# Strassen's product with fifteen sums for the first product of two dense layers, in token groups of 768

## The reference, cut to what matters

```python
# attention with a decaying state: q, k, v are (2, 8, 768, 64)
for t in range(S):
    state = gamma * state + outer(k[t], v[t]);  y[t] = scale * q[t] @ state
x = y as (1536 tokens, 512)
h = x @ w_in                      # (512, 2048)
x = (h * sigmoid(1.702 * h)) @ w_out              # layer 1
xn = x / sqrt(mean(x * x) + 1e-6) * rms_g
x = (silu(xn @ w_gate) * (xn @ w_val)) @ w_out2   # layer 2, 1536 hidden features
```

## Time and profile before

| | us |
|---|---|
| median of 3 runs (lowest, highest) | 622.95 (622.73, 623.17) |
| span of the profiled execution | 621.5 |
| PE busy | 613.0 |
| DVE busy | 338.9 |
| ACT busy | 238.7 |
| POOL busy | 128.7 |

### The profile page before, as it was taken

One profiled execution on the slowest core, in us unless ns is written; L12 is line 12 of the kernel. 1 busy time (PEld: TensorE's weight loads), 2 busy tenths in 40 slices (PEclk: granted clock), 3 DMA queues, 4 the chain that ended last, 5 costly groups with the idle time before them and its releaser, 6 DMA issues.

```text
span 621.5 us, 8409 instructions
## 1 busy us (share of the span) xinstructions
PE 613.0 (99%) x3058; PEld 510.0 (82%) x3058; DVE 338.9 (55%) x463; ACT 238.7 (38%) x407; POOL 128.7 (21%) x98
## 2 busy tenths in 40 slices
PE   7999999999999999999999999999999999999997
PEld 7888888888888888888888888888888888888886
DVE  3665544546644447774446775444755554544443
ACT  1434544444444445444434333333333334332232
POOL 2642000003200006960004970001950000000000
PEclk9999999999999999999999999999999999999999
DMA  8897200000000002323230000001000000100001
GB/s 320 289 403 280 119 0 0 0 0 0 0 0 0 0 1 69 133 62 124 85 137 1 2 0 0 0 0 67 1 0 0 0 0 0 69 0 0 0 1 68
DMA packets 8560, 34.62 MB, mean 56 GB/s; under 512 B 992, under 2 KB 1120, under 8 KB 7520
## 3 DMA queue, kind: packets, MB, share of 16 engines
q1 hardware_dynamic: 8544, 34.42, 15.4%
HBM read 31.27 MB, written 3.15 MB: 55 GB/s over the span
## 4 chain that ended last, share of the span: by engine, by line
PE 95%; DMA 2%; issue 1%; POOL 0%; SPq 0%; DVE 0%; POOLq 0%
PE acc L311 37%; PE gate L311 37%; PE val L311 16%; DMA raw<-attn_in 2%; PE gate L279 1%; PE val L258 1%; PE acc L248 1%; PE gate L273 1%; PE gate L367 0%; PE gate L395 0%; POOL arena L719 0%; POOL arena L711 0%; DVE arena L696 0%; SPq L176 0%; SPq L174 0%
## 5 line engine op out<-in xcount | busy, mean ns | idle before, releaser
L467 ACT ACTIVATE sig<-gate 128x512 f32<-128x512 f32 x83 | 49.6, 597 | 215.6 <-PE val L311 126.8
L311 PE MATMUL gate<-x_hi,win_hi 128*128 128x512 f32 x336 | 130.8, 389 | 0.0
L311 PE MATMUL gate<-x_lo,win_hi 128*128 128x512 f32 x336 | 130.7, 389 | 0.0
L311 PE MATMUL gate<-x_hi,win_lo 128*128 128x512 f32 x336 | 130.7, 389 | 0.0
L625 DVE TENSOR_TENSOR g_lo<-g,g_hi 128x512 fp32r<-128x512 f32 x83 | 63.8, 768 | 58.0 <-ACT g_hi L472 58.0
L587 DVE TENSOR_TENSOR win_lo<-raw,win_hi 128x512 fp32r<-128x512 f32 (+1 forms) x84 | 86.9, 1035 | 11.2 <-ACT win_hi L423 11.2
L472 ACT ACTIVATE g_hi<-g 128x512 fp32r<-128x512 f32 x83 | 52.5, 633 | 96.9 <-DVE g L620 55.8
L593 DVE TENSOR_TENSOR wout_lo<-raw,wout_hi 128x512 fp32r<-128x512 f32 x84 | 69.2, 824 | 16.3 <-ACT wout_hi L427 15.9
L311 PE MATMUL acc<-g_hi,wout_hi 128*128 128x512 f32 x192 | 75.3, 392 | 0.0
L311 PE MATMUL acc<-g_lo,wout_hi 128*128 128x512 f32 x192 | 74.8, 389 | 0.0
L311 PE MATMUL acc<-g_hi,wout_lo 128*128 128x512 f32 x192 | 74.7, 389 | 0.0
(11 more groups left out here) (63 smaller groups left out, 728.1 us busy)
## 6 DMA issues: line engine op xcount, KB each, us to landing
raw<-attn_in SPq DMA_DIRECT2D x24, 512.0 KB, 7.3
raw<-w SPq DMA_DIRECT2D x12, 768.0 KB, 4.2
raw<-w SPq DMA_DIRECT2D x8, 1024.0 KB, 8.6
out<-arena SPq DMA_DIRECT2D x2, 1024.0 KB, 4.5
out<-arena SPq DMA_DIRECT2D x4, 256.0 KB, 2.1
arena<-tables SPq DMA_DIRECT2D x1, 518.0 KB, 5.5
arena<-tables SPq DMA_DIRECT2D x1, 256.0 KB, 7.8
ident<-ident_in SPq DMA_DIRECT2D x1, 64.0 KB, 9.8
```

The source lines that it names most:

```text
L311: mm = pe.matmul(out_ap, a, b, start=start and i == 0, stop=stop and i == len(pairs) - 1)
L467: act.activation(sig[par][:, :], gate[par][:, :], ACT.Sigmoid, scale=1.702 if layer == 1 else 1.0).then_inc(sig_done, 1)
```

## The change

The layers are rewritten; attention keeps its steps, but its output goes to `x32` in full float32, one buffer per batch row, and is split into upper and lower parts later.

- Tokens go in two groups of 768 in place of three blocks of 512. There are four phases: layer 1 for either group, then layer 2 for either group.
- The first product of a layer is taken for two hidden tiles (256 features) by 768 tokens by 512 input features at a time, as a 2 by 2 by 2 block product by Strassen's scheme with seven block products and fifteen sums (Winograd's form). A unit `hidden(p, j)` is seven products, each of 2 feature blocks by 3 passes, so 6 matmuls of 384 columns. Some sums are formed in PSUM by letting several products add into one bank; others by ACT copies and DVE additions (`copy_m1`, `copy_m5`, `copy_u2`, `c12`, `c22`).
- Product 4 of unit `n` adds to what `c22(n)` left, and is issued in the next unit behind that one's products 1 and 5 (`fourth`).
- POOL forms four sums of weight blocks for each unit (`weight_sums`), DVE four sums of input blocks for each phase (`sum_x`). Seven weight blocks and seven input blocks are then split, where four were before.
- All activated features of a group stay on chip (`g32`), and a stage after the hidden stage multiplies them by the second weights into eight banks of 384 columns (layer 1) or six of 512 (layer 2).
- Weights are loaded anew in each phase, 512 KB a unit, through three buffers `raw`.
- The sigmoid followed by a multiplication is replaced by one ACT function in layer 1 and by Silu in layer 2.
- The norm moves from POOL to ACT (squares), DVE (sums, diagonals, `normalise`) and PE, within the hidden stage of the phase that follows.
- The hardware loops are gone; all instructions are written out.

The core of the new code, in the order of engines PE, ACT, DVE, POOL (`lower_next(r, k)` on DVE and `split_next(r, k)` on ACT are parts 0, 1, 2 of the next unit's weights, of 768, 512 and 512 columns, or one part of 1024 for a projection unit; `gate_tile` is the product of Silu and value in layer 2; parts 0, 1 and 2 on ACT wait for 1, 2 and 4 of the unit's POOL sums):

```diff
+HALF = SEQ // 2
+OPERAND = 2 * HALF
+PHASES = ((1, 0), (1, 1), (2, 0), (2, 1))
+HIDDEN = {1: NF1 // 2, 2: NF2}
+PROJECT = {1: NF1 // 2, 2: NF2 // 2}
+SET = ((0, 1, 2), (3, 4, 5))
+FIRST = {1: (6, 7, 0, 1, 2, 4, 3, 5), 2: (6, 7, 0, 1, 2, 4)}
+FINAL = {1: (0, 1, 2, 3, 4, 5, 6, 7), 2: (0, 1, 2, 4, 6, 7)}
...
+def product(i, n, role, half, place, c, start):
+    p, j = hidden_units[n]
+    r = at["hidden", p, j]
+    q = (quad_at[r] + half) % 3
+    dst = bank[SET[n % 2][role]][:, 0:HALF]
+    if j == 0:
+        pe.wait_ge(x_lo_done, 7 * p + c + 1)
+    for kk in range(2):
+        w, x = cols(2 * place + kk, P), cols(2 * c + kk, HALF)
+        pe.matmul(dst, w_hi[q][:, w], x_hi[:, x], start=start and kk == 0, stop=False,
+                  skip_group_check=True)
+        pe.matmul(dst, w_hi[q][:, w], x_lo[:, x], start=False, stop=False, skip_group_check=True)
+        mm = pe.matmul(dst, w_lo[q][:, w], x_hi[:, x], start=False, stop=kk == 1, skip_group_check=True)
+    mm.then_inc(m_done[i], 1)
...
+def fourth(n):
+    pe.wait_ge(c22_done, n + 1)
+    product(4, n, 2, 1, 1, T4, False)
...
+def hidden(p, j):
+    n, r = h_at[p, j], at["hidden", p, j]
+    pe.wait_ge(w_lo_done, lo_at[r] + 1)
+    if n < 2:
+        when(pe, bank_free(n, 2))
+        pe.wait_ge(x_lo_done, 1)
+        pe.matmul(bank[SET[n][2]][:, 0:HALF], w_hi[quad_at[r] % 3][:, 0:P], x_hi[:, 0:HALF],
+                  start=True, stop=True, skip_group_check=True)
+    when(pe, bank_free(n, 0))
+    product(1, n, 0, 0, 1, B11, True)
+    when(pe, bank_free(n, 1))
+    product(5, n, 1, 0, 0, T1, True)
+    if j > 0:
+        fourth(n - 1)
+    pe.wait_ge(w_lo_done, lo_at[r] + 3)
+    pe.wait_ge(m1_copied, n + 1)
+    product(6, n, 2, 1, 2, T2, False)
+    product(2, n, 0, 0, 2, B21, False)
+    pe.wait_ge(m5_copied, n + 1)
+    product(3, n, 1, 1, 3, B22, False)
+    pe.wait_ge(u2_copied, n + 1)
+    product(7, n, 2, 1, 0, T3, False)
...
+def norm_bcast(i):
+    pe.wait_ge(mean_done, i + 1)
+    pe.wait_ge(diag_done, i + 1)
+    for th in range(2):
+        mm = pe.matmul(bank[6 + th][:, 0:HALF], ones[:, :], diag[:, cols(th, HALF)], start=True, stop=True)
+    mm.then_inc(bcast_done, 1)
...
+for p, (layer, _) in enumerate(PHASES):
+    for j in range(HIDDEN[layer]):
+        hidden(p, j)
+        if p in (1, 2) and j == 2:
+            norm_totals(p - 1)
+        if p in (1, 2) and j == 4:
+            norm_bcast(p - 1)
+    project_phase(p)
...
+def copy_m1(n):
+    act.wait_ge(m_done[1], n + 1)
+    when(act, bank_free(n, 2))
+    a, b = SET[n % 2][0], SET[n % 2][2]
+    act.activation(bank[b][:, 0:HALF], bank[a][:, 0:HALF], ACT.Copy).then_inc(m1_copied, 1)
...
+def squares(i, th):
+    if th == 0:
+        act.wait_ge(evac_act, evac_at[i + 1])
+        act.wait_ge(evac_dve, evac_at[i + 1])
+    if 2 * i + th > 0:
+        act.wait_ge(sum_sq_done, 2 * i + th)
+    for dh in range(2):
+        act.activation(square[dh][:, :], x32[i][:, cols(2 * dh + th, OPERAND)], ACT.Square)\
+           .then_inc(squared, 1)
...
+for c in (T1, T2, B22, T3, T4):
+    split_x(0, c)
+for p, (layer, _) in enumerate(PHASES):
+    for j in range(HIDDEN[layer]):
+        n, r = h_at[p, j], at["hidden", p, j]
+        if j > 0 and not is_val(n - 1):
+            activate(n - 1, 2)
+        copy_m1(n)
+        copy_m5(n)
+        if j > 0 and not is_val(n - 1):
+            activate(n - 1, 3)
+        split_next(r, 0)
+        copy_u2(n)
+        if not is_val(n):
+            activate(n, 0)
+        split_next(r, 1)
+        split_next(r, 2)
+        if not is_val(n):
+            activate(n, 1)
+        if p in (1, 2) and j < 2:
+            squares(p - 1, j)
+        if j == HIDDEN[layer] - 1:
+            split_g(p, 0)
+            split_g(p, 1)
+    for j in range(PROJECT[layer]):
+        n, r = h_at[p, HIDDEN[layer] - 1], at["project", p, j]
+        if j == 0 and not is_val(n):
+            activate(n, 2)
+        split_next(r, 0)
+        for f in (2 * j + 2, 2 * j + 3):
+            if f < TILES[layer]:
+                split_g(p, f)
+            if f == 2 and not is_val(n):
+                activate(n, 3)
+        if p < len(PHASES) - 1 and 1 <= j <= 4:
+            for c in ((B11, B21), (T1, T2), (B22, T3), (T4,))[j - 1]:
+                split_x(p + 1, c)
+        split_next(r, 1)
+        split_next(r, 2)
...
+def sum_x(i, c):
+    g = PHASES[i][1]
+    b11, b12, b21, b22 = (x_block(g, b) for b in (B11, T1, B21, B22))
+    if c == T1:
+        if i < 2:
+            dve.wait_ge(y_copied, 11 + i)
+        else:
+            dve.wait_ge(x_normed, 8 * (i - 1))
+        dve.wait_ge(x_lo_done, 7 * i + 1)
+        dve.tensor_tensor(t3[:, :], b22, b12, ALU.subtract).then_inc(x_sums, 1)
+        dve.tensor_tensor(b12, b12, b11, ALU.subtract).then_inc(x_sums, 1)
+    elif c == T2:
+        dve.wait_ge(x_sums, 4 * i + 2)
+        dve.tensor_tensor(b11, t3[:, :], b11, ALU.add).then_inc(x_sums, 1)
+    else:
+        dve.wait_ge(x_sums, 4 * i + 3)
+        dve.wait_ge(x_lo_done, 7 * i + 2)
+        dve.tensor_tensor(b21, b21, b11, ALU.subtract).then_inc(x_sums, 1)
...
+def c12(n):
+    b = bank[SET[n % 2][1]][:, 0:HALF]
+    dve.wait_ge(m_done[3], n + 1)
+    dve.wait_ge(u2_copied, n + 1)
+    dve.tensor_tensor(b, b, u2[n % 2], ALU.add).then_inc(c12_done, 1)
...
+def c22(n):
+    a, b = bank[SET[n % 2][0]][:, 0:HALF], bank[SET[n % 2][2]][:, 0:HALF]
+    dve.wait_ge(m_done[7], n + 1)
+    dve.wait_ge(m5_copied, n + 1)
+    dve.wait_ge(*taken(n, 1))
+    dve.tensor_tensor(a, b, m5[n % 2], ALU.add).then_inc(c22_done, 1)
...
+def add_squares(i, th):
+    dve.wait_ge(squared, 4 * i + 2 * th + 2)
+    dve.tensor_tensor(square[0][:, :], square[0][:, :], square[1][:, :], ALU.add).then_inc(sq_added, 1)
+    if i > 0 and th == 0:
+        dve.wait_ge(total_done, i)
+    dve.wait_ge(sq_added, 2 * i + th + 1)
+    dve.tensor_tensor(sum_sq[:, cols(th, HALF)], square[0][:, 0:HALF], square[0][:, HALF:OPERAND],
+                      ALU.add).then_inc(sum_sq_done, 1)
...
+def normalise(i, th):
+    dve.wait_ge(bcast_done, i + 1)
+    for k in range(KT):
+        x = x_tile(i, k, th)
+        dve.scalar_tensor_tensor(x, x, gain[:, k:k + 1], bank[6 + th][:, 0:HALF], ALU.mult, ALU.mult)\
+           .then_inc(x_normed, 1)
...
+    if s == 8:
+        lower_x(0, B11)
+        lower_x(0, B21)
+    if s == 10:
+        lower_w(0, 0)
+        lower_w(0, 1)
+lower_w(0, 2)
+sum_x(0, T1)
+lower_x(0, T1)
+sum_x(0, T2)
+lower_x(0, T2)
+lower_x(0, B22)
+lower_x(0, T3)
+sum_x(0, T4)
+lower_x(0, T4)
+for p, (layer, _) in enumerate(PHASES):
+    for j in range(HIDDEN[layer]):
+        n, r = h_at[p, j], at["hidden", p, j]
+        if j > 0:
+            c22(n - 1)
+            if is_val(n - 1):
+                gate_tile(n - 1, 2)
+                gate_tile(n - 1, 3)
+        lower_next(r, 0)
+        if is_val(n):
+            gate_tile(n, 0)
+        lower_next(r, 1)
+        c12(n)
+        if is_val(n):
+            gate_tile(n, 1)
+        lower_next(r, 2)
+        if p in (1, 2):
+            if j < 2:
+                add_squares(p - 1, j)
+            if j == 3:
+                means(p - 1)
+            if j == 4:
+                diagonals(p - 1)
+            if j in (5, 6):
+                normalise(p - 1, j - 5)
+        if j == HIDDEN[layer] - 1:
+            lower_g(p, 0)
+            lower_g(p, 1)
...
+def weight_sums(r):
+    a11, a12, a21, a22 = (raw[r % 3][:, cols(k, 256)] for k in range(1, 5))
+    s1 = raw[r % 3][:, 0:256]
+    pool.wait_ge(raw_in[r % 3], 16 * (r // 3) + 16)
+    pool.tensor_tensor(s1, a21, a22, ALU.add).then_inc(w_sums, 1)
+    pool.wait_ge(w_sums, sums_at[r] + 1)
+    pool.tensor_tensor(a21, a11, a21, ALU.subtract).then_inc(w_sums, 1)
+    pool.wait_ge(w_lo_done, lo_at[r] + 1)
+    pool.wait_ge(w_sums, sums_at[r] + 2)
+    pool.tensor_tensor(a11, s1, a11, ALU.subtract).then_inc(w_sums, 1)
+    pool.wait_ge(w_sums, sums_at[r] + 3)
+    pool.tensor_tensor(a12, a12, a11, ALU.subtract).then_inc(w_sums, 1)
...
+for r, (kind, p, j) in enumerate(units):
+    if kind == "hidden":
+        weight_sums(r)
+        if p in (1, 2) and j == 5:
+            pool.wait_ge(half_set, 1)
+            pool.wait_ge(mean_done, p)
+            pool.tensor_tensor(inv_rms[:, :], mean_sq[:, :], minus_half[:, :], ALU.pow)\
+                .then_inc(inv_done, 1)
...
```

More of the change, by code:

```diff
@@ L84, in part @@
             return arena[:, used[0] - cols:used[0]]
+        slot = [part(2048) for _ in range(SLOTS)]
         table = part(T_ALL)
@@ L158, in transformer_kernel @@
-        loads += [(i * RAW2, RAW2, w2, i * RAW2) for i in range(NF2)]
-        def raw_count(n):
-            if n < NF1:
-                return n // 2 + 1
-            if n < N1:
-                return NF1 // 2
-            return NF1 // 2 + min(n - N1, NF2 - 1) + 1
+        stored = [sem(f"stored{i}") for i in range(BATCH)]
+        units = []
+        for p, (layer, _) in enumerate(PHASES):
```

(39 more changed lines are left out.)

891 lines of the change are left out of this document (401 added, 490 removed).

## The result

The changed kernel takes 646.22 us (median of 4 runs, 644.24 to 649.68) against 623.06 (622.73 to 623.33) before: a ratio of 1.0376, 95% interval 1.034 to 1.0412. It is slower, as forecast (633.0, range 614 to 660, 0.73 for slower), but by 3.8% where 1.6% was forecast, and above the 645 at which the forecast's own case ended. The profiled execution took 644.55, with a span of 642.8, which is 11.1 above the forecast span of 631.7.

A forecast was written before the change was run, and what follows sets the result against it. PE was taken as the bound, busy 613.0 of 621.5 us. Start 66.4 + 2.0, matmuls 522.4 + 0.3, waits and norm 10.9 + 7.0 + 4.0 + 7.3 + 6.5 + 1.3, tail 3.6: 631.7; with 1.45, 633, range 614 to 660.

The forecast's parts named there:

- cheaper matmuls: PE in the layers: matmuls of 384 columns pay less than 0.0134 us extra; at 0.005, 612 us; chance 0.22.
- weight loads: PE: weight loads can't run beside the matmul before; 0.27 us per 384 columns, over 800 us; chance 0.03.
- The start: First unit, behind attention: layers start in effect at 66.4 us against 57.34, plus 2.0 for half clock.
- the squares: Units 0 and 1 of phases 1 and 2: `c22` waits behind the norm's squares; 10.9 us together.
- the wait for the diagonals: Norm's broadcast behind unit 4: PE waits for DVE's diagonals, held up by POOL's power; 3.5 us twice, 7.0.
- the passage to the projections: Hidden stage to projection: PE waits for the first tile's split and lowering; 2.1, 2.1, 1.15, 1.15, together 6.5 us.
- Silu's table load: ACT, ahead of the first unit's activation: one load, 1.28 us, entered as 1.3 in the sum.
- bounds 0 and 4, I take 2: First unit's work behind two idle stretches of PE: 4 us more at 1.2 GHz if the clock falls; 2 taken.
- I cost the steady units at zero stall: Steady units: layer 1's chain to `c22` ends at 7.24 us against PE's 7.28; no wait was added.
- The rival that named it: Steady units bound by POOL and DVE: 8 us per 0.1 on a sum; chance 0.20 for more than 645.
- Normalise: Units 5 and 6: four DVE instructions ahead of `c22`; waits of 1.9, 1.9, 1.9, 1.6, together 7.3 us.
- The totals: Norm's matmuls on PE: six totals at 0.7 us, twice, within the 4.0 us for the norm's matmuls.

The follow-up runs named there:

- `c22` first: DVE runs `c22` ahead of weights part 2, squares, diagonals and normalise: on the changed kernel 625.07 us; undone in the version with all orders 625.44 us.
- the kernel kept busy: Changed kernel plus 25 and 26 unused matmuls ahead of products 5 and 6 of the first unit: 643.73 us.
- the version with all orders: Changed kernel with start order, `c22`, norm broadcast and first tile's split moved, squares spread over units 1 and 2, totals moved: 596.98 us.
- the later POOL: Changed kernel with POOL's first sum of a unit waiting until DVE has lowered the unit before: 652.07 us.
- the three tried both ways: `c22` first, later broadcast, start's order: each alone on the changed kernel (625.07, 641.86, 642.92 us), each undone in the version with all orders (625.44, 609.09, 602.74).
- after: The changed kernel itself, without any follow-up edit, against the kernel before: 646.22 us, ratio 1.0376.
- with the clock held up: The version with all orders plus 13 and 8 unused matmuls in the first unit's two waits: 596.50 us.
- all but the later broadcast: The version with all orders, but the norm's broadcast again behind unit 4 instead of behind product 3 of unit 5: 609.09 us.

## Why the prediction was right in direction and short in size

Right was the frame: PE's work shrinks by 32 and waits plus a late start take up more. The pace (0.1734 forecast, 0.1733 measured) settles the rivals of cheaper matmuls and of weight loads. The start (68.4 against 67.4), the squares, the wait for the diagonals and the passage to the projections lie within 1.0 each, at the places named. Two of these hold partly by luck: of the four waits behind squares three are within 0.3 (3.2, 3.1 and, with the table load, 3.8), but the last took 1.3 where 2.4 was forecast; and the broadcast is taken up below. `c22` first, alone and taken away again, shows that DVE's order is the cause, not its amount of work: it was busy for 348.4 us with the waits and 353.0 without. Silu's table load took 1.28 and ACT's next instruction began at 347.49, 0.01 behind its end, so nothing followed the load. (The Trainium skill, ScalarE: Activation LUTs, "What ACT_TABLE_LOAD costs", has a drain behind it, 1.4 more by the prediction's estimate; this trace does not agree.)

The 11.1 that were missing in the span are mis-sized terms, three above all. The step that failed is pricing PE's waits by their length alone, with no half clock behind them and nothing for a chain without slack:

- **Half clock, "bounds 0 and 4, I take 2", and only at the start.** The 2 held there: 2.4 of it lay on PE's path, by the kernel kept busy. But 4.6 more came behind the squares of layer 2's first unit and behind both broadcasts, where the prediction named waits of 2.7 with 1.3 for the table load, and of 3.5 twice, and gave them no clock price. The norm's four broadcast matmuls and the restart behind them took 2.84 and 2.85 at half clock; in the version with all orders, at full clock, 1.30, exactly the 1.3 forecast.
- **"I cost the steady units at zero stall".** The chain was found to equal PE's time, 7.24 against 7.28, and zero was taken. Layer 1 ran at 7.44, layer 2's pairs at 14.81 instead of 14.56: 3.4 in all. `c22` was late by about 0.03 in layer 1 and 0.13 in layer 2, and each of these waits cost 0.11 more at the restart: the first two matmuls start 0.28 apart (82.46 and 82.74 in the trace of the later POOL) where 0.17 is usual. A chain with no slack should have had a price. The rival that named it, with more than 645 as its place, had the rule: 0.3 a unit for each 0.1 on a POOL sum. A sum took 0.74 against 0.69, and the rule then gives 4.2 over 28 units. In the steady unit above two sums end 5.23 behind the issue of product 4 where 5.02 was forecast: 0.1 of that is in the sums, and the other 0.1 was there before them, since ACT's activation 3 waits for product 4, which PE's restart delays. So that rival's mechanism was at work, at a third of the excess, and the time of 646.22 lies at its place only together with the clock.
- **"Normalise" and the means.** 8.9 and 0.9 against 7.3 and 0: the same short slack, since all that was put ahead of `c22` was counted against PE's 7.28 without restarts and with DVE's part 2 at its earliest. How the 2.5 divides between these is not shown.

The totals add 1.3 (2.7 against 1.4: six of them came as twelve matmuls in 1.25, not 0.7). POOL's power took 1.79 for six columns against 1.42 for four, and six diagonals 2.12 against the 1.2 taken from the earlier trace rows; both lie inside the broadcast's wait. That wait came out within 0.7 by luck: the prediction had the power hold up DVE's part 2, which it did not, so the diagonals began 0.4 earlier than forecast (7.1 behind the issue of product 4 against 7.5), and then took 0.9 longer.

The median lies a further 1.7 above the profiled run. The runs differ in their clock, but which waits were followed by a slow stretch in the longer ones I can't say, since they have no profile.

## What to carry to other kernels

A result that the bottleneck engine waits for should stand in each engine's order by when it is needed; here a handful of moved calls turned +3.8% into -4.3% with the same instructions. Before an algorithm that saves arithmetic is judged, let its waits be taken out: this one's gain of 32 us was hidden by its order. Test orders together and by taking them away from the best version, since singly they understate (for waits alone, 27.7 against 37.0 us for the three tried both ways). Count each wait of PE with its restart and its clock, and where the clock differs from run to run, look at the waits before a difference of a few us is put down to an edit.

## What the hardware showed that was not expected

- Each restart of PE behind `c22` costs 0.11 us, also where the wait was only 0.03: the 23 stops about 2.5 us by that. Behind ACT's copy of product 1 the first two matmuls start 0.25 apart, so 0.08 (the version with `c22` first, 204.41).
- POOL's power of 128 x 6 elements, 1.79 long, did not keep out a DVE subtraction of two SBUF operands (0.68 at 239.80, inside it, and 0.67 the second time), though its sums do.
- The granted clock fell to 1.2 GHz in or behind waits of 3.6 to 4.4 us after, and in the profile of the kernel kept busy at the start also at places where after has none (windows of that kernel):

```profile
125.00:129.00 4.00, 3.27 (x14) 0.78 0.11 38
203.00:208.00 5.00, 2.11 (x8) 0.77 0.37 105
```

  After ran these stretches, behind waits of 2.1 and 3.1 us, at full clock. So runs of one kernel with many such waits differ: 5.4 us between the fastest and slowest after, 0.8 with all orders, 0.2 with the clock held up. Long waits alone need not do it: all but the later broadcast has two of about 4 us and its runs differ by 0.8.
- Diagonals (one operand of 128 columns in SBUF and a scalar for each partition) take 0.27 each and up to 0.74 when POOL works in SBUF: the exclusion of the earlier trace rows reaches such DVE instructions too. In the version with all orders two POOL sums of 0.95 and 0.80 lie beside six diagonals that take 2.22 us together.
